# Retention scores and values computed in half chunks of keys, on quarters of the array

## The reference, cut to what matters

```python
# q, k, v: (8 batches, 8 heads, 576 positions, 64)
scores = (1 / sqrt(64)) * q @ k.T
Dmat   = where(rel >= 0, gamma[h] ** rel, 0)     # rel = query position - key position
x      = (scores * Dmat) @ v                     # (8, 8, 576, 64), then (4608 tokens, 512)
h      = max(x @ w1, x @ w2, x @ w3)             # d_ff 768
x      = h @ w_out
out    = ((x @ u1) * (x @ u2)) @ u3 @ u_out      # d_ff 1024
```

## Time and profile before

| | |
|---|---|
| median of 3 runs | 1220.27 us |
| the profiled execution | 1221.08 us |
| its span, first to last instruction | 1219.2 us |
| TensorE busy | 1209.0 us, 99% |
| first part ends (first L1268) | 165.75 us |
| a repeating step of the first part (m = 6 to 10) | 9.31 us |
| granted TensorE clock in the first part | 1.00 |

### The profile page before, as it was taken

How to read it: one execution, slowest core, us unless ns; L and a number is a source line. 1 busy time by engine, 2 the same in 40 slices (tenths; PEclk the granted TensorE clock), 3 DMA queues, 4 the chain that set the end, 5 groups by cost and what they waited for, 6 DMA issues and landing times.

```text
span 1219.2 us, 21648 instructions
## 1 busy us (share of the span) xinstructions
PE 1209.0 (99%) x8594; PEld 1190.1 (98%) x8594; DVE 739.5 (61%) x1065; ACT 487.5 (40%) x781; POOL 431.8 (35%) x234
## 2 busy tenths in 40 slices
PE   8999999999999999999999999999999999999999
PEld 8898899999999999999999999999999999999998
DVE  5555747746454454658887777454545456876652
ACT  3444544423232322326655444232424234554451
POOL 3645645220202010063787660202020217465550
PEclk9999999999999999999999999999999999999999
DMA  9999943021212030234554541313121252444441
GB/s 346 332 364 376 322 141 134 33 85 46 78 46 85 26 105 27 73 136 147 179 218 170 169 139 53 110 52 110 60 104 64 99 189 89 155 157 161 162 156 65
DMA packets 87332, 169.55 MB, mean 139 GB/s; under 512 B 9272, under 2 KB 58680, under 8 KB 87232
## 3 DMA queue, kind: packets, MB, share of 16 engines
q1 hardware_dynamic: 87232, 168.17, 39.2%
HBM read 106.27 MB, written 61.87 MB: 138 GB/s over the span
## 4 chain that ended last, share of the span: by engine, by line
PE 92%; DMA 3%; SPq 2%; DVE 1%; issue 1%; ACT 0%; POOL 0%; ACTq 0%; DVEq 0%; POOLq 0%
PE ps L1268 28%; PE ps L1270 28%; PE ps L1269 28%; PE ps L1177 2%; PE ps L1120 1%; PE ps L1192 1%; PE ps L1165 1%; PE ps L1194 1%; PE ps L1196 1%; PE ps L1140 1%; DMA vs<-vv 1%; DMA qks<-qk 1%; DMA xd<-xst 1%; DMA hd<-h 1%; DVE probs L952 0%
## 5 line engine op out<-in xcount | busy, mean ns | idle before, releaser
L1268 PE MATMUL ps<-chi,whi 128*128 128x384 f32 x2016 | 673.9, 334 | 0.9 <-ACT w L931 0.6
L1270 PE MATMUL ps<-chi,wlo 128*128 128x384 f32 x2016 | 673.5, 334 | 0.0
L1269 PE MATMUL ps<-clo,whi 128*128 128x384 f32 x2016 | 673.4, 334 | 0.0
L674 POOL TENSOR_TENSOR raw<-raw,raw 128x768 f32<-128x768 f32 (+3 forms) x102 | 267.8, 2646 | 582.7 <-DMA raw<-xd 203.6
L1268 PEld LDWEIGHTS ps<-chi,whi 128*128 128x128 f32 x2016 | 378.4, 188 | 2.1 <-ACT w L931 1.0
L1269 PEld LDWEIGHTS ps<-clo,whi 128*128 128x128 f32 x2016 | 378.5, 188 | 0.0
L1270 PEld LDWEIGHTS ps<-chi,wlo 128*128 128x128 f32 x2016 | 378.4, 188 | 0.0
L940 DVE TENSOR_TENSOR clo<-raw,chi 128x768 fp32r<-128x768 f32 (+2 forms) x168 | 253.2, 1535 | 29.6 <-ACT chi L851 29.5
L851 ACT CAST chi<-raw 128x768 fp32r<-128x768 f32 (+2 forms) x168 | 180.3, 1081 | 83.8 <-PE ps L1270 54.7
L931 ACT COPY w<-ps 128x384 f32<-128x384 f32 x126 | 60.6, 481 | 240.6 <-PE ps L1270 239.0
L918 ACT COPY u<-ps 128x384 f32<-128x384 f32 x126 | 60.6, 481 | 160.6 <-PE ps L1270 159.0
(11 more groups left out here) (61 smaller groups left out, 796.0 us busy)
## 6 DMA issues: line engine op xcount, KB each, us to landing
gd<-h SPq DMA_DIRECT2D x96, 192.0 KB, 1.9
raw<-gd SPq DMA_DIRECT2D x24, 768.0 KB, 6.4
qks<-qk SPq DMA_DIRECT2D x30, 576.0 KB, 7.4
hd<-h SPq DMA_DIRECT2D x72, 192.0 KB, 1.9
raw<-hd SPq DMA_DIRECT2D x24, 576.0 KB, 6.0
x2d<-h SPq DMA_DIRECT2D x48, 192.0 KB, 2.2
raw<-x2d SPq DMA_DIRECT2D x24, 384.0 KB, 4.2
outT<-h SPq DMA_DIRECT2D x48, 192.0 KB, 1.9
```

Source lines behind the costliest of these rows:

```text
L674: return nc.gpsimd.tensor_tensor(out_, a, b, op)
L1268: nc.tensor.matmul(to, w1, x1, start=(start and k == 0), stop=False, skip_group_check=True)
L1269: nc.tensor.matmul(to, w1, x2, start=False, stop=False, skip_group_check=True)
L1270: last = nc.tensor.matmul(to, w2, x1, start=False, stop=(k == KH[st] - 1), skip_group_check=True)
```

## The change

Scores and values no longer compute the quarter of each 128x128 chunk that the mask makes zero (first 64 queries with last 64 keys).

1. Keys are taken in halves of 64, so a score matmul uses a quarter of the array. Which half of the output rows a half of the keys goes to is swapped for odd n (`key_rows`), and the host lays out values, keys and tables accordingly. From step 2 on (`SINGLE`) both pairs of a step are scored together (`scores_of_two`): four matmuls for a chunk and half, 128 queries for the first half of the keys, 64 for the second. In steps 0 and 1 `scores` still covers all 128 queries. The tail uses 64 keys.
2. Values are split: `values_of_halves` takes the first 64 queries of each chunk with the first 64 keys, and the tail, four matmuls beside each other; `values` takes the last 64 queries with all 128 keys.
3. `sum_state` moves to the end of the step, behind the values. `SUMS_FIRST` and its wait are gone.
4. `scores_of_two` waits for the loads of both pairs and for `x_out` of both. VectorE decays the first heads of both pairs, then the second heads. `query_states` waits for the first heads only, and for the second ahead of its last chunk (`decayed_heads`).
5. The tail of v has a tile of its own, loaded in one piece for two pairs; ten memsets at the start and the wait for them are gone. The mask table has two variants.

```diff
-SUMS_FIRST = (4, 5)
+SINGLE = 2
+def key_rows(n, half):
+    return slice((half ^ n % 2) * DH, (half ^ n % 2) * DH + DH)
+def decayed_heads(m, all_heads):
+    return min(3 * NP, 6 * m + (4 if all_heads else 3 if m < SINGLE else 2))
...
+                else:
+                    for h in range(2):
+                        for n in made_in(m):
+                            decay_scores(n, h)
...
+            def scores_of(n, c, half, first_query):
+                for h in range(2):
+                    own = slice(h * DH, h * DH + DH)
+                    keys = SEQ + c * CH + half * DH
+                    nc.tensor.matmul(ps[key_rows(n, half), 2 * (n % 2) + h, c * CH + first_query:(c + 1) * CH],
+                                     rows_of(n)[own, keys:keys + DH],
+                                     rows_of(n)[own, c * CH + first_query:(c + 1) * CH], ...)
+            def scores_of_two(first):
+                pair = (first, first + 1)
+                for n in pair:
+                    pe.wait_ge(qk_loaded[rows_sem(n)], rows_count(n))
+                pe.wait_ge(decayed, 3 * first)
+                pe.wait_ge(x_out, first - 2)
+                for c in range(NC):
+                    for half in range(2):
+                        for n in pair:
+                            scores_of(n, c, half, half * DH)
+                for n in pair:
+                    tail_scores(n)
...
-                pe.wait_ge(decayed, min(3 * (first + 2) + 4, 3 * NP))
+                pe.wait_ge(decayed, decayed_heads(first // 2 + 1, False))
                 for c in range(1, NC + 1):
+                    if c == NC:
+                        pe.wait_ge(decayed, decayed_heads(first // 2 + 1, True))
...
+            def values_of_halves(first):
+                pe.wait_ge(decayed, 3 * (first + 2))
+                pe.wait_ge(queried, first + 2)
+                pe.wait_ge(vt_loaded[first // 2 % 3], 16 * (first // 6 + 1))
+                for c in range(NC):
+                    for n in pair:
+                        rows = key_rows(n, 0)
+                        for h in range(2):
+                            nc.tensor.matmul(ps[out_rows(n, h), 2 * (n % 2), c * CH:c * CH + DH],
+                                             vs[rows, n % 6, c * P + h * DH:c * P + h * DH + DH],
+                                             probs[n % 4][rows, h, c * CH:c * CH + DH], ...)
+                ... (the tail: 64 key rows, 64 queries)
...
-                for n in made_in(m):
-                    if n in SUMS_FIRST:
-                        sum_state(n)
                 if m:
                     query_states(2 * m - 2)
-                for n in made_in(m) if m else ():
-                    if n not in SUMS_FIRST:
-                        sum_state(n)
+                    values_of_halves(2 * m - 2)
                 for n in read_in(m):
                     values(n)
+                for n in made_in(m) if m else ():
+                    sum_state(n)
```

More of the change, by code:

```diff
@@ L339, in build @@
         v_at = comb_base[B] + 4 * 6144
[L340 to L341 removed]
+        vs = at("vs", [P, 6, NC * CH], f32, v_at)
+        vtail = at("vtail", [P, 3, P], f32, v_at + 6 * NC * CH * 4)
+        ks = [at(f"ks{i}", [P, K_COLS], f32, (v_at + 6 * NC * CH * 4 + 3 * P * 4, o)[i]) for i in range(2)]
         ks_first = [at(f"ks_first{i}", [P, K_COLS], f32, 26112 + i * K_COLS * 4) for i in range(4)]
@@ L1113, in scores @@
                     pe.wait_ge(qtab_made, 1)
-                if n >= 4:
-                    pe.wait_ge(x_out, n - 3)
                 for c in range(NC):
[L1117 to L1128, removed]
+                    for half in range(2):
+                        scores_of(n, c, half, 0)
+                tail_scores(n)
[6 more added lines that the diff above has]
+                for c in range(NC):
+                    for half in range(2):
+                        for n in pair:
+                            scores_of(n, c, half, half * DH)
+                for n in pair:
+                    tail_scores(n)
             def sum_state(n):
@@ L1169, in query_states @@
                             last.then_inc(queried, 1)
+            def values_of_halves(first):
+                pair = (first, first + 1)
+                pe.wait_ge(decayed, 3 * (first + 2))
[4 more added lines that the diff above has]
+                        rows = key_rows(n, 0)
+                        for h in range(2):
+                            nc.tensor.matmul(ps[out_rows(n, h), 2 * (n % 2), c * CH:c * CH + DH],
+                                             vs[rows, n % 6, c * P + h * DH:c * P + h * DH + DH],
+                                             probs[n % 4][rows, h, c * CH:c * CH + DH],
+                                             start=False, stop=False, skip_group_check=True)
+                for n in pair:
+                    rows = key_rows(n, 1)
+                    for h in range(2):
+                        nc.tensor.matmul(ps[out_rows(n, h), 2 * (n % 2) + 1, 0:TAIL],
+                                         vtail[rows, n // 2 % 3, h * DH:h * DH + DH],
+                                         probs[n % 4][rows, h, NC * CH:SEQ],
+                                         start=False, stop=True, skip_group_check=True)
@@ L1171, in values @@
             def values(n):
[L1172 to L1175, removed]
+                for c in range(NC):
                     for h in range(2):
-                        last = nc.tensor.matmul(ps[out_rows(n, h), bank, cols], vs[:, n % 6, c * P + h * DH:c * P + h * DH + DH],
-                                                probs[n % 4][:, h, c * CH:min(SEQ, (c + 1) * CH)],
-                                                start=False, stop=(c >= NC - 1), skip_group_check=True)
+                        last = nc.tensor.matmul(ps[out_rows(n, h), 2 * (n % 2), c * CH + DH:(c + 1) * CH],
+                                                vs[:, n % 6, c * P + h * DH:c * P + h * DH + DH],
+                                                probs[n % 4][:, h, c * CH + DH:(c + 1) * CH],
+                                                start=False, stop=(c == NC - 1), skip_group_check=True)
@@ L1222, in _ @@
             run_idle(9, S_WC)
-            pe.wait_ge(zeroed, 10)
             for m in range(STEPS):
-                for n in made_in(m):
+                if m >= SINGLE and made_in(m):
+                    scores_of_two(2 * m)
+                for n in made_in(m) if m < SINGLE else ():
                     scores(n)
```

85 lines of the change are left out of this document (44 added, 41 removed).

## The result

The changed kernel took 1247.43 us (median of 4 runs, 1246.62 to 1251.80), the kernel before 1220.48 (4 runs, 1220.11 to 1221.44): a ratio of 1.0227, 95% interval 1.0202 to 1.0251. The forecast was 1214.0, with a range of 1205.5 to 1219.5. The sign was wrong.

What follows compares the result with a forecast made beforehand. The prediction took TensorE as the bound, with DMA engines nearly full and limiting steps 6 to 14. 1221.1 - 0.4 - 4.5 - 1.4 = 1214.8, less 0.8 for the median: 1214.0 us, range 1205.5 to 1219.5.

Steps and rivals of the forecast that it cites:

- the third rival: TensorE's instruction fetch, steps 6 to 14: stalls of 0.3 us a step give back 2.7, 1216.7 us; 9%.
- 4.5 us off in steps 6 to 14: Steps 6 to 14: DMA engines at 384 GB/s need 79.9 us where steps take 84.4, allowing 4.5 off.
- steps of 8.6 to 9.0: Sign of being right: steps 6 to 14 this long in us, TensorE idle ahead of scores, DMA share 1.0.
- TensorE's prices: Blocks of a full step on TensorE: scores 1.66 us, queries 0.83, values 1.66, sums 1.03.
- 8.53 for 8.1: Full step on TensorE: forecast to go from 9.31 to 8.1 us, 1.2 less.
- the 79.9 of the forecast: Steps 6 to 14: time in us for 30.67 MB at 384 GB/s, where the steps take 84.4.
- Early steps, 0.4 off: Up to step 6: 0.4 us off, with 2.0 off and 1.0 added as the ends.
- The lost cover in step 2: Step 2: queries start at 3.6 us, wait for second heads until 4.9; step takes 7.7, where it took 7.2.
- Steps 15 and 16, 1.4 off: Steps 15 and 16, loads over: TensorE saves 1.2 and 0.5 us, 0.3 goes back for ScalarE's read; 1.4 off.
- The slower rival, late sums: Load loop: late sums delay key and q loads; at 8.5 us landing steps take 10.4, 1228.4 us; 8%.

Runs made afterwards that it cites:

- the undisturbed step above: One step without stalls, wc left out, in the changed kernel with loads from pair 6 on cut to 128 columns: 8.53 us; that run took 1221.47 us.
- short loads: Changed kernel with loads of q and k, v and keys cut to 128 columns from pair 6 on (output not the reference's): 1221.47 us, ratio 1.0000.
- the cross: Loads from pair 6 on cut to 128 columns, in the changed kernel (1221.47 us) and in the kernel before with value matmuls cut in two (1222.23 us).
- whole values: Changed kernel with values over all 128 keys and queries again, scores in halves and sums last kept: 1238.02 us, ratio 1.0141.
- values in two: Kernel before with each value matmul of 128 columns cut into two of 64, same transfers and order: 1232.48 us for 1221.55, ratio 1.0093.

## Why the prediction was wrong

**The step that failed** is in the third rival, "instructions come late": "A stall of 0.3 us in each of nine steps gives back 2.7", with 9%. The mechanism was named, with its two rows, the count of records and the place (140 of them in 3.3 us), and then sized as if the single stall of 1.01 us grew little. (By the prediction's own prices the dense part is 136 records in 3.5 us.) Measured: 19.4 us of stalls for 1.0; 9.8 of them in the nine steps, where I had 2.7, and 9.6 in steps that the rival didn't count. The sum of the forecast has no term for it at all: its 4.5 us off in steps 6 to 14 came out as 13.9 us added. Two things were missed.

- The limit is a rate. From the state queries to the end of the scores the kernel before has 32 + 32 + 40 + 40 = 144 records, 288 instructions with the weight loads, in 6.4 us: a block of 256 in 5.7 us. The changed kernel has 32 + 40 + 32 + 32 + 72 = 208 records, 416 instructions, in 5.6 us by the undisturbed step above: a block in 3.4 us. The one stall in the kernel before showed an edge, and was taken for a rare event.
- The supply goes through the same DMA engines, at a share of 1.0. The rival says so, but nothing was priced from it. The sum took the full DMA engines as a limit for data only, and forecast the stretch at a share of 1.0 with steps of 8.6 to 9.0. With the loads cut, the same instructions came on time.

The Trainium skill, page "Runtime: NRT & Kernel Launch", section "Instruction fetch mechanics", says that blocks of 256 instructions are fetched ahead in sequence while the engine runs, and that this is hidden by the pace of issue. The trace agrees with the 256 (2048 instructions more, 8 packets more) and with one block fetched while another runs. It doesn't agree that it is hidden: 19.4 us were not, with the DMA engines full.

**The other steps.**

- TensorE's prices were right within 0.1 us for each block; the step came to 8.53 for 8.1, mostly because of one term left out: a wait for TensorE's own last query (0.33 a step).
- "So the DMA engines allow 4.5 us off": never reached. In the changed kernel TensorE doesn't wait for q and k once, and the DMA share fell. With short loads the nine steps take 80.3 us, near the 79.9 of the forecast by luck: no limit of data is at work there.
- Early steps, 0.4 off: 10 us lost, of which 3.1 up to step 2. The lost cover in step 2 was priced in the right direction, but restoring it gave nothing; 3.90 us went at 21 us in one stall.
- Steps 15 and 16, 1.4 off: 0.2 lost. The loads are over, but a late block takes 0.8 us of the scores of step 15, the wait for TensorE's own query 0.33 in each step, and the first dense product waits 0.27 for ScalarE's read. No run separates these.
- The slower rival, late sums, had about the right size by luck. It gave 8 us more, and the sums at the end cost 7 us alone, but there TensorE waits on issue and at half clock, and never for q and k. In the change as it is, the x stores are late (6.0 us of TensorE's time); with the stores put first, q and k are (7.9), as the rival said.
- The clock was in no term. It is at 0.50 in four stretches, each behind idle time of TensorE (3.90 us before the first, 2.76 before the second, 2.6 and 2.4 in two pieces before the others), and never in the kernel before. By the rows it costs about 7.4 us. Other idle times of 2.1 us (before 48.03) and of 2.15 and 0.49 (before 81.49 and 82.87) were not followed by a fall. I take the half clock as following from the stalls; no run separates the two.

**By size**, in the first part: late instructions +18.4 us (19.4 for 1.0), x stores +5.7, wait for own queries +2.3 idle, half clock +7.4, and the rest of the idle time +1.5, against 11.2 us of work saved. The first two also follow from each other in part, since a stall shifts loads and stores. These parts are one trace's accounts, not separate experiments. What the runs show is the cross: 26 of 27 us vanish when the transfers shrink, the waits for x stores and 10 of the 17 us at half clock among them. And 10.9 appear in the old kernel when only its instructions grow, of which 10.3 vanish with short loads.

**What stays open.** When a fetch is asked for isn't in the trace, only when its packet starts. So why one packet starts 1.4 us after the block before began and another 5.8 is not settled. Also open is why whole values, with 188 records, stall on issue for only 1.8 us where values in two, with 188, stall for 8.0. The rows say where it lies: with whole values the packets start at most 3.2 us (2.0 on average) after the block before began, with values in two up to 7.0 (3.5 on average). Whole values wait for stores instead, which spaces the blocks, but no run tells whether that is all. The shares of the x stores and of the half clock in the change have no run of their own. None of these kernels beat the one before.

## What to carry to other kernels

Count instructions per microsecond, and not only columns, before cutting matmuls into smaller ones: where a stretch already has an unexplained issue stall and full DMA engines, more and shorter instructions can cost time, though the array does less. Look at the instruction queue as at a load with a due time. If such a cut is wanted, free the DMA engines in that stretch first; and when a producer goes to the end of a step, follow both the loads and the stores queued behind it.

## What the runs showed of the hardware

- TensorE's instructions came in blocks of 256 (16 KB, about 1 us for each packet) through the DMA engines that carry the data, one packet for each block, while the block before it ran. After the packet's end it took 1.25 to 1.6 us until a waiting TensorE went on.
- With whole loads (a DMA share of 0.93 to 1.02 in steps 6 to 14) these packets started 2.2 to 3.5 us after TensorE began the block before, on average in the kernel before, the changed one and the one with values in two; with short loads (0.55 to 0.58) 0.7 to 1.7 us.
- The longest stall, 3.9 us, came at a share of 1.05 (16.0 to 22.3 us). In steps 6 to 14 of the changed kernel, at 0.93, the longest on issue was 1.75 us, and with short loads 1.1.
- Loads of half the length at the same bytes brought the packets 0.2 to 0.4 us earlier on average (one profile of each kernel), with the longest stall again at 3.9 us.
- Behind idle times of 2.76 and 3.90 us the granted clock fell to 0.50, its level of 1.2 GHz, and stayed there for 3.4 and 6.8 us.
